# Three unrolled loops of a three-part kernel rewritten as hardware loops: TensorE, VectorE and ScalarE

## What is computed

```python
for t in range(S):                       # the attention part, one (40 x 40) state for each head
    m_new = np.maximum(f_gate[:, :, t] + m, i_gate[:, :, t])
    f_stab, i_stab = np.exp(f_gate[:, :, t] + m - m_new), np.exp(i_gate[:, :, t] - m_new)
    m = m_new
    C = f_stab[:, :, None, None] * C + i_stab[:, :, None, None] * np.einsum('bhd,bhe->bhde', vt, kt)
    n = f_stab[:, :, None] * n + i_stab[:, :, None] * kt
    y[:, :, t] = sigmoid(o_gate[:, :, t]) * (C @ qt) / max(abs(n @ qt), 1)
x = y as 3072 rows of 320
h = x @ w_in;  x = np.maximum(0.01 * h, h) @ w_out       # MLP 1
h = x @ w2_in; out = (h * np.cos(h)) @ w2_out            # MLP 2
```

## Time and profile before

| | us |
|---|---|
| median of three runs | 871.83 |
| lowest and highest | 870.23, 872.74 |
| the profiled execution | 872.74 |
| span in the profile, first to last instruction | 870.9 |

### The profile page before, as it was taken

How to read it: one execution, slowest core, us unless ns; L and a number is a source line. 1 busy time by engine, 2 the same in 40 slices (tenths; PEclk the granted TensorE clock), 3 DMA queues, 4 the chain that set the end, 5 groups by cost and what they waited for, 6 DMA issues and landing times.

```text
span 870.9 us, 15491 instructions
## 1 busy us (share of the span) xinstructions
PE 850.9 (98%) x5766; PEld 836.0 (96%) x5766; DVE 651.0 (75%) x1177; ACT 463.4 (53%) x1015; POOL 305.2 (35%) x302
## 2 busy tenths in 40 slices
PE   8999999999999999999999999999999999999997
PEld 8889999998999999999999999999999999999997
DVE  6999687577577676685864468888888888888885
ACT  5155433423432333433424677777777777777775
POOL 5664624114033032222100664333333333333333
PEclk9999999999999999999999999999999999999999
DMA  7383704322322323243202340201010101010000
GB/s 245 103 271 98 234 15 154 129 77 91 129 84 84 129 88 119 90 166 130 68 2 91 122 169 1 94 20 50 19 49 21 47 23 46 24 45 24 2 23 23
DMA packets 30840, 74.08 MB, mean 85 GB/s; under 512 B 3121, under 2 KB 16945, under 8 KB 30769
## 3 DMA queue, kind: packets, MB, share of 16 engines
q1 hardware_dynamic: 30720, 73.07, 24.5%
q10 hardware_dynamic: 48, 0.05, 0.0%
HBM read 61.11 MB, written 11.99 MB: 84 GB/s over the span
## 4 chain that ended last, share of the span: by engine, by line
PE 58%; issue 24%; POOL 13%; DVE 3%; ACT 1%; POOLq 0%; ACTq 0%
PE h L556 21%; POOL g_lo L1235 13%; PE acc L566 7%; PE acc L568 7%; PE acc L567 7%; PE x L533 4%; PE s L482 3%; PE x L520 2%; PE s L508 2%; PE x L540 2%; PE s L556 1%; PE acc L628 1%; PE acc L636 1%; DVE x L940 0%; DVE g_lo L980 0%
## 5 line engine op out<-in xcount | busy, mean ns | idle before, releaser
L556 PE MATMUL h<-xT,w_in 128*128 128x384 f32 x1536 | 302.5, 339 | 1.3 <-DVE xT L972 1.3
L682 ACT ACTIVATE t_f<-h 128x384 f32<-128x384 f32 x192 | 94.2, 491 | 326.9 <-PE h L556 326.9
L556 PEld LDWEIGHTS h<-xT,w_in 128*128 128x128 f32 x1536 | 266.5, 188 | 1.6 <-DVE xT L972 1.6
L566 PE MATMUL acc<-w_out,g_hi 128*128 128x320 f32 x768 | 245.1, 319 | 4.3 <-POOL g_lo L1235 4.3
L568 PE MATMUL acc<-w_out,g_lo 128*128 128x320 f32 x768 | 238.0, 310 | 0.0
L567 PE MATMUL acc<-w_out,g_hi 128*128 128x320 f32 x768 | 237.0, 309 | 0.0
L1235 POOL TENSOR_TENSOR g_lo<-g_f,g_hi 128x384 fp32r<-128x384 f32 x128 | 131.7, 1029 | 213.2 <-ACT g_hi L682 213.2
L566 PEld LDWEIGHTS acc<-w_out,g_hi 128*128 128x128 f32 x768 | 144.9, 189 | 8.3 <-POOL g_lo L1235 3.1
L567 PEld LDWEIGHTS acc<-w_out,g_hi 128*128 128x128 f32 x768 | 145.0, 189 | 0.0
L568 PEld LDWEIGHTS acc<-w_out,g_lo 128*128 128x128 f32 x768 | 144.6, 188 | 0.0
L987 DVE TENSOR_TENSOR g_f<-h,t_f 128x384 f32<-128x384 f32 x128 | 71.0, 555 | 96.3 <-ACT t_f L682 95.3
(11 more groups left out here) (127 smaller groups left out, 874.5 us busy)
## 6 DMA issues: line engine op xcount, KB each, us to landing
qk_s<-qk SPq DMA_DIRECT2D x24, 512.0 KB, 3.8
kvo_s<-kvo SPq DMA_DIRECT2D x24, 484.0 KB, 4.8
D<-g_dram SPq DMA_DIRECT2D x21, 512.0 KB, 5.5
x_dram<-stage SPq DMA_DIRECT2D x8, 960.0 KB, 4.7
xT<-x_dram SPq DMA_DIRECT2D x8, 960.0 KB, 4.8
eG_b<-e_dram SPq DMA_DIRECT2D x46, 128.0 KB, 5.4
out<-x SPq DMA_DIRECT2D x24, 160.0 KB, 1.8
raw_in<-w1i SPq DMA_DIRECT2D x8, 384.0 KB, 5.1
```

The costliest lines, as they stand in the source:

```text
L556: last = nc.tensor.matmul(bank[:, 0:BLOCK], w(a), x[:, k, :], start=(n == 0), stop=(n == 7))
L566: nc.tensor.matmul(acc[t][:, 0:DM], g_hi[:, s, r], w_out[:, 0, j, :], start=(j == 0), stop=False)
L682: copy = lambda o, i, **k: nc.scalar.activation(o, i, ACT.Copy, **k)
```

## The change

`over_the_row` gets the engine as its first argument, and its two loops of three turns become hardware loops (`engine.Fori`) on PE, ACT and DVE. The instruction stream then holds one turn of each loop, which runs three times: a counter in a register, an addition and a compare-and-branch at the end of the body, and the branch goes back twice and falls through once. Inside the body every wait whose count depends on `b` compares with a register, and register instructions ahead of it work the count out. The order of the work and the work itself are the same, and POOL's and SP's code is the same.

```diff
-        def over_the_row(slot):
+        def over_the_row(engine, slot):
             for i in range(FT + LAG):
                 slot(Row(0, 0, 0), i)
-            for b in range(BATCH - 1):
+            with engine.Fori(0, BATCH - 1) as b:
                 for i in range(LAG, 2 * FT + LAG):
                     slot(Row(b * 2 + 1, 1, b), i)
             for i in range(LAG, 2 * FT + LAG):
                 slot(Row(BLOCKS - 1, 1, BATCH - 1), i)
-            for b in range(BATCH - 1):
+            with engine.Fori(0, BATCH - 1) as b:
                 for i in range(LAG, 2 * FT + LAG):
                     slot(Row(b * 2 + (BLOCKS + 1), 1, None, True), i)
             for i in range(LAG, FT + LAG):
                 slot(Row(2 * BLOCKS - 1, 1, None, True), i)
...
-            over_the_row(slot)
+            over_the_row(pe, slot)
...
-            over_the_row(slot)
+            over_the_row(act, slot)
...
-            over_the_row(slot)
+            over_the_row(dve, slot)
```

## The result

The changed kernel takes **882.13 us** in the median of four runs (881.54 to 882.53), beside 872.16 for the kernel before (four runs, 870.23 to 872.74). The ratio is 1.0117, with a 95% interval of 1.010 to 1.0135: slower by 10 us, where 876.9 (871.0 to 882.0) was predicted. In every group of runs the ratio compares executions at the undisturbed clock alone, so it isn't always the quotient of the two medians beside it. The profiled execution took 883.32 us, with a span of 881.6 beside 870.9 before.

A forecast was written before the change was run, and what follows sets the result against it. PE, busy 98% of the span, was taken to bound the kernel; 0.3 us of register work, 0.8 in the first loop and 4.0 in the second sum to 5.1, making 871.83 into 876.9 us, range 871.0 to 882.0.

The forecast's parts named there:

- What bounds the kernel: Whole kernel: PE bounds it, busy 98% of the span, nobody else above 75%; only holes in PE's stream change the time.
- PE has 3.0 and 1.7 us in hand: Where branches go back: PE's sequencer reads ahead 3.0 us in the first loop, 1.7 in the second; only longer stalls cost.
- Register work 0.3 us: Both loops: added register instructions cost 0.3 us (0 to 1.5), at places where PE waits for the transposed tile.
- entering and falling out, nothing: Start and end of the loops: both go on to the next instruction, the branch takes 45 ns, so no cost.
- I take it that it isn't: Branches back: the old packet with the body's head is no longer there, so the branch waits for a transfer.
- The stall, 3.2 us (1.4 to 6.2): Each branch back: 1.8 us transfer, 1.2 for PE's packet, 0.2 for branch and resumption; bounds 1.4 and 6.2 us.
- The queue of instructions has no other transfer ahead of it: Refetch at a branch back: reason for taking a transfer time near the quick kind's 1.8 us, not the slowest's 6.0.
- The sums: Both loops, two branches back each: 0.4 us each in the first (0.8), 2.0 us each in the second (4.0).
- Code still held: Rival, branches back: old packets are still there, branches cost 0.1 to 0.2 us, time 872.1 us; chance 0.34.
- A stall is much dearer: Rival, branches back: second transfer or attention inputs make stalls 5.5 to 6 us, 15 us in all, 887 us; chance 0.14.
- The register work shows in every slot: Rival, MLP 2: register instructions take 0.9 us a slot, some 0.1 us of 96 slots is PE's, 882 us; chance 0.04.
- The signs named ahead of the run: PE holes near 229, 353 (close to nothing), 652, 741 us (1.5 us), releaser "issue"; packets about as before; other MLP 2 slots 2.73 us.

The follow-up runs named there:

- e_spread8: Changed kernel with first loop unrolled and PE's second body spread by jumps over 8 packets of 256, head at a packet's start: 881.22 us, ratio 1.0109.
- e_second_only: Changed kernel with the first loop unrolled again, the second kept as a hardware loop on PE, ACT and DVE: 870.49 us, ratio 1.000.
- e_act_dve_only: Changed kernel with hardware loops on ACT and DVE alone, PE's turns written out: 872.85 us, ratio 1.0013.
- e_hint: Changed kernel plus a prefetch hint for the back branch on PE at the head of each loop body: 870.37 us, ratio 1.0005.
- e_spread7: Like the 8-packet spread of PE's second body, first loop unrolled, but with six jumps instead of seven, so 7 packets: 873.37 us, ratio 1.0001.
- e_fit64: Changed kernel with PE's first body cut to 1,791 instructions, head at place 64 of a packet, reaching an eighth packet: 892.63 us in one run, total not used.
- e_fit0: Changed kernel with PE's first body cut to 1,791 instructions (one wait for acc), head at a packet's start, filling 7 packets: 870.23 us, ratio 1.0005.
- e_pe_only: Changed kernel with hardware loops on PE alone, ACT's and DVE's turns written out: 882.97 us, ratio 1.0147.
- e_swap: Changed kernel with SP's load of the next chunk put ahead of the store of x2: 877.42 us, ratio 1.0065.

## Why the prediction was wrong, point by point

**What bounds the kernel; PE has 3.0 and 1.7 us in hand.** Right. PE went on for 2.9 us behind the first branch, and for 1.8 us in the second loop of e_spread8. That part of the method can be trusted: the distance between the sequencer's row and the engine's row at the place is what a stall may last for nothing.

**Register work 0.3 us; entering and falling out, nothing.** Right within what can be measured: the second loop, which has most of it on ACT, took 261.76 us instead of 261.80, and the ratios of e_second_only, e_act_dve_only and e_hint are 1.000, 1.0013 and 1.0005. (Entering costs something only where the head is placed at a packet's start and a jump leads there: the holes of 2.77 and 3.33 us of e_spread8 and e_spread7.)

**"I take it that it isn't" there any more.** This is the step that failed, for five of the six bodies. The prediction treated all bodies alike and gave the other answer a rival's chance for all of them alike. The runs show a capacity. PE loses the head of a body that reaches properly into an eighth packet (e_fit64, e_spread8) and keeps one of seven (e_fit0, e_spread7). So it holds about eight packets of 256 instructions, the one fetched ahead included. The second body, at 4.5 packets, is far inside that. ACT and DVE kept bodies of 278 and 270 instructions; how much more they hold no run shows. The packets in the first loop follow: the three turns of after fetch 7, 9 and 9, together 25, where the same slots unrolled take 21 (e_second_only).

The section "Instruction fetch mechanics" of the page "Runtime: NRT & Kernel Launch" of the Trainium skill gives TensorE room for 2,048 instructions, eight such packets; that agrees with where the stall begins here. The same section says that only two pages are held and that a branch out of them waits. Here the traces disagree: PE went back 1,162 instructions, 4.5 packets, in 0.22 us. The prediction had both statements and gave all bodies one answer; dividing each body by the larger one would have put 1,794 instructions and the packet fetched ahead at its edge, and the others far inside.

**The stall, 3.2 us (1.4 to 6.2).** For quiet DMA engines this was close: 3.35 to 3.64 us measured, in e_spread8. In part this is luck: of its terms 1.8 + 1.2 + 0.2 us the packet's 1.2 is right (0.95 and 1.28), but the rest is 1.0 us until the packet starts and 1.35 us from its end to the branch's. The mis-sized part is the first loop, 5.9 us. "The queue of instructions has no other transfer ahead of it" is true of its own queue, not of the 16 DMA engines that it shares with SP's transfers. The mean share of 0.28 in the loop's window hid that it is 1.02 at this place. The kernel before has the same burst there, 0.83 to 1.03 between 222 and 230 us, and the windows would have shown it.

**The sums.** First loop: 0.8 us expected for both places; the two slots grew from 2.73 us to 6.11 and 6.05 (slot 2 of block 3: first products at 228.28 and 234.39), 6.7 us in all. 5.9 - 2.9 = 3.0, with 0.2 us from the branch to the first matmul, is the prediction's own formula with the right stall in it. Second loop: 4.0 expected, 0 measured; where a stall was forced on PE there, its holes were 2.0 and 1.7 us, beside 1.5 forecast for PE. That the forecast was 2.0 in all is no hit: the other 0.4 to 0.5 us were to come from a stall of ACT, and ACT had none.

**What the prediction didn't have: the clock.** A hole of 3.2 us was followed by the lower clock in one of two places of after and in both of e_pe_only, 1.6 us each. But a fall needs no stalled branch: each of the two profiled executions has one more in its first loop, behind two short waits at the attention products (0.80 and 0.50 us in before, 0.73 and 0.43 in after). First before, which the earlier trace rows rounds to 1.00, then after (PE busy, granted clock, DMA share, GB/s):

```profile
268.70:272.10 3.40, 3.40 (x16) 0.50 0.00 0
147.50:150.90 3.40, 3.40 (x15) 0.50 0.15 37
```

These two cancel, so between the profiled executions one fall more is left, and 6.7 + 1.6 = 8.3 of the 9.4 us of the first loop are accounted for. The last 1.1 us stay open. PE's waits at the attention products aren't it, as they are 7.0 us in before and 6.9 in after. In e_pe_only they are longer. PE's waits in the stretch 107 to 480 us, in e_pe_only and in e_hint, which ran beside it:

```profile
PE h L566 <- issue: 6.3, 2, 3.2
PE x L530 <- issue: 5.0, 9, 1.3
PE s L518 <- DVE D L923: 1.3, 2, 0.7
```

```profile
PE x L524 <- issue: 3.5, 8, 0.5
PE s L512 <- DVE D L917: 0.7, 1, 0.7
```

Beside the 6.3 us of the two holes there are 2.1 us more at the attention products (L530 and L518 there are L524 and L512 in e_hint). With 3.2 us of clock that is 11.6 of the 11.8 us by which the loop of e_pe_only is longer (373.9 and 362.1). Whether the stall has to do with that isn't shown: this wait at L520 in the numbering of after was between 3.0 and 7.4 us in all runs, with a stall and without.

**The rivals.** "Code still held" was right for five of the six loop bodies and had the time wrong only through the sixth. "A stall is much dearer", 5.5 to 6 us behind the transfers of the attention inputs, named the mechanism and the size of what happened in the first loop (2.5 to 3 us of hole each; measured 3.2), and was wrong about the second. The time, 882.1, lies at the lower edge of its 882 to 890, for this mixed reason. "The register work shows in every slot" has 882 too, and there the agreement is luck: the slots of MLP 2, in which it should show, took 261.76 us, as before. The signs named ahead of the run were the right ones: packets, holes at "issue", equal slots in MLP 2. Of these the holes near 229 and 353 us were there, those near 652 and 741 were not.

## What to carry to other kernels

Before a loop is rolled up, count its body in instructions for each engine (on PE every matmul counts at least twice, as weight load and matmul) and compare it with what the engine holds. On PE here seven packets of 256 go back in 0.2 us, and eight cost 3.5 us with quiet DMA engines and up to 6.9 with busy ones. Where the body lies counts as well as its length: at the limit, 1,794 instructions stalled, and with a prefetch hint or with the head at a packet's start they didn't. With the hint, or with the head placed and three instructions less, the loop cost nothing that could be measured. What a stall costs is its length less what the engine has in hand at that place, and its length must be read with the DMA share of that very microsecond, not with the loop's mean.

## What the runs showed of the hardware that I had not expected

- The prefetch hint acts on what is kept: with it the packet behind the body isn't fetched ahead (six packets in the first turn instead of seven), and PE fetched nothing for 266 us (203 to 469), though its body of about 1,795 instructions reaches an eighth packet wherever its head lies.
- A packet of instructions is held up by data on another queue: it started 1.0 us after the branch that wanted it on quiet DMA engines, and 3.4 us after it at a share of 1.02. The branch ended another 1.3 to 1.5 us after the packet did, in all six cases of the table.
- ACT went back over 278 instructions in 50 ns and DVE over 270 in 67 ns, although their instructions come in packets of half the size.
- Behind the four holes of 3.2 us in after and in the kernel with loops on PE alone, TensorE came back at 1.2 GHz three times, at 1.6 us each. Behind 2.8, 2.0 and 1.7 us in e_spread8 it kept 2.4 GHz; behind the 2.1 us in e_swap, and behind waits of at most 0.8 us in before and after, it didn't. The length of a hole alone doesn't tell which it will be.
